# Block 0 of a dense stage: where the low parts of the next weights are made, and which of them the gate products wait for

## What is computed

```python
# 1. linear attention with a decaying state, 4 batches, 8 heads of 48
for t in range(768):
    cur = einsum('bhd,bhe->bhde', u * k_t, v_t)
    y[t] = einsum('bhd,bhde->bhe', r_t, state + cur)
    state = w * state + einsum('bhd,bhe->bhde', k_t, v_t)
# 2. dense gated layer, d_ff = 1536
g = x @ w_gate
x = ((g * sigmoid(g)) * (x @ w_val)) @ w_out
# 3. eight experts of width 1024, one for each token
e = argmax(x @ w_gate2)
out = p[e] * sigmoid(x @ w_output_gate)[e] * (relu(x @ w1[e]) @ w2[e])
```

## Time and profile before

| | |
|---|---|
| median of 3 runs | 837.93 us |
| profiled execution, own time | 837.9 us |
| its span | 836.1 us |
| TensorE busy | 819.7 us (98%) |
| VectorE busy | 484.4 us (58%) |
| ScalarE busy | 368.0 us (44%) |
| GpSimd busy | 200.7 us (24%) |
| granted clock of TensorE, mean | 0.998 |

### The profile page before, as it was taken

How to read it: one execution, slowest core, us unless ns; L and a number is a source line. 1 busy time by engine, 2 the same in 40 slices (tenths; PEclk the granted TensorE clock), 3 DMA queues, 4 the chain that set the end, 5 groups by cost and what they waited for, 6 DMA issues and landing times.

```text
span 836.1 us, 19906 instructions
## 1 busy us (share of the span) xinstructions
PE 819.7 (98%) x7825; PEld 719.0 (86%) x7825; DVE 484.4 (58%) x1004; ACT 368.0 (44%) x703; POOL 200.7 (24%) x159
## 2 busy tenths in 40 slices
PE   6999999999999999999999999999999999999996
PEld 4777788888888888888888888899999999999996
DVE  7767644335543454435343443469968877897771
ACT  3644333223332243324332322456566776687661
POOL 3434205331354043502420210003111111111010
PEclk9999999999999999999999999999999999999999
DMA  8455203111221022202200116057997668776700
GB/s 335 159 169 171 70 8 115 62 60 40 88 95 61 10 90 86 97 1 97 87 1 2 39 39 243 23 214 233 339 391 260 249 244 298 289 248 249 284 18 19
DMA packets 24146, 116.72 MB, mean 140 GB/s; under 512 B 3372, under 2 KB 9824, under 8 KB 18448
## 3 DMA queue, kind: packets, MB, share of 16 engines
q1 hardware_dynamic: 19984, 101.16, 34.1%
q0 software_dynamic: 3520, 9.87, 3.1%
q10 hardware_dynamic: 576, 4.72, 1.6%
HBM read 102.64 MB, written 14.16 MB: 140 GB/s over the span
## 4 chain that ended last, share of the span: by engine, by line
PE 90%; DVE 3%; ACT 1%; issue 1%; POOLq 0%; DVEq 0%; ACTq 0%
PE bank L1727 33%; PE bank L1774 6%; PE bank L1776 5%; PE bank L1775 5%; PE bank L1847 5%; PE bank L1849 5%; PE bank L1848 5%; PE bank L1812 3%; PE bank L1814 3%; PE bank L1813 3%; PE bank L1808 3%; DVE WL L1135 2%; PE bank L1654 1%; PE bank L1788 1%; PE bank L1809 1%; PE bank L1608 1%
## 5 line engine op out<-in xcount | busy, mean ns | idle before, releaser
L1727 PE MATMUL bank<-X1H,WH 128*128 128x512 f32 x432 | 169.2, 392 | 2.0 <-DVE WL L1135 2.0
L1727 PE MATMUL bank<-X1L,WH 128*128 128x512 f32 x432 | 168.0, 390 | 0.0
L1727 PE MATMUL bank<-X1H,WL 128*128 128x512 f32 x432 | 168.0, 390 | 0.0
L1318 DVE TENSOR_TENSOR PP<-SG,bank 128x512 f32<-128x512 f32 (+1 forms) x78 | 49.9, 646 | 201.8 <-PE bank L1727 186.2
L760 ACT ACTIVATE AH<-PP 128x512 fp32r<-128x512 f32 (+1 forms) x78 | 46.0, 597 | 167.2 <-DVE PP L1318 167.2
L865 ACT ACTIVATE SG<-bank 128x512 f32<-128x512 f32 x72 | 42.9, 596 | 139.2 <-PE bank L1727 136.5
L1727 PEld LDWEIGHTS bank<-X1H,WH 128*128 128x128 f32 x432 | 81.0, 188 | 20.7 <-DVE WL L1135 3.7
L1727 PEld LDWEIGHTS bank<-X1H,WL 128*128 128x128 f32 x432 | 81.0, 188 | 17.4 <-DVE WL L1135 0.3
L1727 PEld LDWEIGHTS bank<-X1L,WH 128*128 128x128 f32 x432 | 81.0, 188 | 16.7 <-DVE X1L L1141 0.3
L1774 PE MATMUL bank<-AH,WH 128*128 128x512 f32 (+1 forms) x234 | 92.4, 395 | 0.0
L743 POOL DMA_INDIRECT out<-YO,IDX x31 | 38.3, 1234 | 218.3 <-ACT YO L955 209.4
(11 more groups left out here) (236 smaller groups left out, 1825.8 us busy)
## 6 DMA issues: line engine op xcount, KB each, us to landing
W_EVEN<-w SPq DMA_DIRECT2D x20, 1536.0 KB
W_ODD<-w SPq DMA_DIRECT2D x18, 1536.0 KB, 7.7
RK_IN<-unit_rk SPq DMA_DIRECT2D x19, 736.0 KB, 5.5
V_IN<-unit_v SPq DMA_DIRECT2D x20, 480.0 KB, 3.5
STG<-w_dense ACTq DMA_DIRECT2D x4, 1152.0 KB, 5.2
XG_ODD<-store SPq DMA_DIRECT2D x9, 394.0 KB, 8.4
store<-PAD SPq DMA_DIRECT2D x8, 394.0 KB
STG<-w_dense SPq DMA_DIRECT2D x2, 1152.0 KB, 9.2
```

Source lines behind the costliest of these rows:

```text
L1318: return tt(PP[:, part], SG[:, part], VALUE_PS[:, part], ALU.mult)
L1727: last = mm(bank_[:, :], lhs[:, f, m, k * P:k * P + P], rhs[:, k, :], start=(x == 0), stop=(x == len(terms) - 1))
```

## The change

Two lines are changed. VectorE makes the three low parts of pair f // 2 + 1 at the end of the odd step f instead of at the end of the even step. And TensorE's gate product of an even step f waits only for the first of the three parts, where it waited for all three; each odd step now has a wait for all three parts of its own pair, which only step 1 had.

```diff
                     if first:
-                        if f % 2 == 0 and f // 2 + 1 < PIECES:
+                        if f % 2 == 1 and f // 2 + 1 < PIECES:
                             dense_lows(f // 2 + 1)
...
-                    if first and (f == 1 or (f and f % 2 == 0)):
-                        pe.wait_ge(dense_low, 3 * (f // 2) + 3)
+                    if first and f:
+                        pe.wait_ge(dense_low, 3 * (f // 2) + (3 if f % 2 else 1))
```

## The result

The changed kernel takes 841.94 us (median of 6 executions, 840.91 to 842.93), the kernel before 837.86 (6 executions). The ratio is 1.0049, with a 95% interval of 1.0039 to 1.0059: slower by 4.1 us, 3.3 to 4.9. The profiled execution took 840.91 us with a span of 839.1, 3.0 us more than before. A second series, beside other kernels, gave a ratio of 1.0041 (1.0028 to 1.0055).

The account below looks back on a forecast made before the run. TensorE, busy 98% of the span, was taken as the bound, so its gaps decide. +1.65 + 0.06 + 1.38 = +3.09 us, rest nothing, gave span 839.2 and 841.0 us; range 839.3 to 842.4, the forecast's own 840.2 to 841.8.

Parts of the forecast that it names:

- Gate 2: TensorE's gate product of step 2: first WL follows SG, PP, AL and the addition of step 1; starts 1.65 us later.
- Gates 4, 6, 8: Gate products of steps 4, 6, 8: WL waits behind RW, leaving gaps of 0.61 us each; sum +0.06 us.
- case 3: Steps 3, 5, 7: WL and RW both run slowly side by side, gaps 1.08 us each; 842.4 us, chance 0.07.
- Gate 10: Gate product of step 10: waits for WL, now behind AL of step 9; +1.27 and 0.11 restart, +1.38 us.
- Everything else at nothing: Rest of block 0: later second and third WL, STG load, SG and odd-step waits cost nothing.
- Rival 1: Steps 3, 5, 7: WL goes first or is never blocked by RW; sum +0.93, 838.8 us, chance 0.10.
- Rival 2: Later in TensorE's work: slack, a DMA above all, absorbs the loss; at best 836.1 us, chance 0.06.
- Rival 4: TensorE behind the larger gap at step 2: clock falls to 1.2 GHz, another 4 us, 845 us, chance 0.03.

Follow-up runs that it names:

- both ends back: The changed kernel, but the WL of pairs 1 and 5 are made in steps 0 and 8 again: 837.57 us, ratio to the kernel before 0.9988.

## Why the prediction was right, point by point

The forecast was 841.0 us, and 839.2 for the profiled span. The profiled execution took 840.91, with a span of 839.1. The median of six is 841.94, inside the stated range of 839.3 to 842.4, but above the 840.2 to 841.8 that I gave the forecast itself.

- *Gate 2, +1.65.* Measured by starts, the gap was 2.33 against 0.83: +1.50. The mechanism was right: PP waits for SG (39.14 against 39.29 forecast), and WL follows behind PP, AL and the addition. Putting pair 1 back took 2.6 us of span, the sum forecast for it, and moving SG moved the gate. The gate came 0.22 earlier than forecast: SG was 0.15 earlier in this execution (38.48 against 38.63 before), and AL stood 1.38 behind PP instead of 1.44. TensorE itself was 0.07 earlier, which leaves the 0.15.
- *Gates 4, 6, 8, +0.06.* The forecast was a gap of 0.61 each, and 0.61, 0.62 and 0.61 were measured. The port was judged rightly from two rows: the end of WL 0.81 behind RW, measured 0.83. Without RW the first WL is short again; with WL issued first, GpSimd waits. The Trainium skill, "SBUF — State Buffer", section "SBUF: two separate sides", gives an exclusive lock held for the whole instruction and taken by the one that starts first; the traces here agree (1406 ns behind RW in the changed kernel, 945 to 960 alone there and with the first part ahead of AL). Shared bandwidth, my case 3, is out.
- *Gate 10, +1.38.* The measured gap is 1.28, and a restart comes to it: +1.39.
- *Everything else at nothing.* This was right. ScalarE's split of pair 5 waited 0.93 us for its load, and SG of step 9 was still in time, as worked out.
- *Rival 1* (WL not blocked) did not come true: RW started 1.09 us ahead of WL in step 3. The kernel with the first part ahead of AL makes it true by another way, and there it is worth more than I gave it, since the early WL relieves gates 2 and 10 too.
- *Rival 2* (absorbed later) did not come true: span and block 0 agree within 0.1 us, so nothing is absorbed.
- *Rival 4, the clock, 0.03.* This was sized wrongly. The question I asked was whether the clock falls in every execution, and the answer is no; but it very likely falls in about a third of them. I took the clock of the stretch with a gap of 0.8 us as evidence for one of 2.5, and the rows held no gap of that size in the middle of the work. The price of 4 us was too high: a fall cost about 1.5 us in the kernel with the move alone and about 1.8 in the one without RW. A third of the executions with such a loss explains part of the distance between +3.1 forecast and +3.5 to +4.1 measured, and the scatter of the experts' stage may explain more; how much each does stays open.

That the sum met the profiled span within 0.1 us is in part luck: the second trace of the same kernel has 840.0. What the prediction worked out is the difference made in block 0, and there both traces bear it out, with 3.02 and 3.08 us of dense stretch for the 3.09 of the sum.

The rows also held a thing that I read and did not use: the second and third WL of a pair took 3.9 us behind the first in steps 2, 4 and 6 and 2.8 in step 0, which is more than any of the gaps, so the relaxed wait alone would close all four. The best two versions, 835.24 and 835.51 us, both beat the kernel before by 0.33 to 0.35%, and can't be told apart.

## What to carry to other kernels

When a change has two edits, price each alone on the same rows: here the waits alone took 3.3 us off the dense stretch, and the move on top of them put 6.3 on. Moving work out of a step relieves only who waits for it there; look for the first consumer, and count the chain in front of the work in its new place, in the first and the last step above all, where the neighbours differ. If a wait can't be avoided, put the part that is waited for into a slot where its engine idles anyway (here between PP and AL), ahead of what competes for the same port. And compare stretches that the edit can reach: here the start and the experts' stage differed by more, from one execution to the next, than some of the edits were worth.

## What was not expected of the hardware

TensorE's granted clock fell to its lower level behind idle stretches of about 2 us at one time and not at another. In the traces it fell behind gaps of 4.02, 2.20, 2.20 and 2.85 us of the kernel with the move alone, behind the 2.22 us at gate 2 without RW, and behind the 2.04 us in the experts' stage with both ends back. It did not fall behind a third gap of 2.20 us of the kernel with the move alone, nor behind the 2.18 and 2.24 us in the two traces of the changed kernel. Behind 2.04 us the experts' stage took 3.8 us longer than its shortest, which is the wait and about 1.8 us more.

The mean clocks agree with this as far as they go. A mean clock below 0.997 came in 9 of 27 executions with a gap of 2.2 us in block 0, and in none of the 12 with that gap filled by nine matmuls. It came in none of the 12 executions of the kernel whose largest gap in block 0 is 1.34 us, the 12 with one of 1.12 or the 8 with one of 0.44. One of 13 with both ends back had it, and its fall is the one in the experts' stage. Of the 68 executions of the kernel before that ran beside the experiments, one had it too; it was not profiled, and where its fall lies is open.
